# A three-stage attention and MLP kernel: two unrolled loops rolled up, a load moved behind other loads, and two copies moved one place ahead

## The reference

```python
# q, k, v: (8, 8, 576, 64), float32
scores = scale * np.matmul(q_c, k_c.transpose(0, 1, 2, 4, 3))     # in chunks of 64 tokens
attn = np.exp(scores - np.max(scores, axis=-1, keepdims=True))
attn = attn / (np.sum(attn, axis=-1, keepdims=True) + 1e-09)
x = np.matmul(attn, v_c)                                          # then (4608 tokens, 512)
h = x @ w_in_a;  r = np.maximum(h, 0.0);  y = (r * r) @ w_out_a   # first MLP: 512 -> 2048 -> 512
h = y @ w_in_b                                                    # second MLP, same sizes
g = np.where(h >= 1, h, np.where(h <= -1, 0.0, (h + 1) ** 2 / 4))
out = g @ w_out_b
```

## Time and profile before

| | us |
|---|---|
| median of 3 runs | 1613.38 (1612.52 to 1613.61) |
| the profiled execution's own time | 1612.52 |
| its span in the profile | 1610.7 |
| PE busy (matmuls) | 1599.8, 99% of the span |
| DVE busy | 1069.9, 66% |
| ACT busy | 628.8, 39% |
| POOL busy | 229.3, 14% |

### The profile page before, as it was taken

One profiled execution on the slowest core, in us unless ns is written; L12 is line 12 of the kernel. 1 busy time (PEld: TensorE's weight loads), 2 busy tenths in 40 slices (PEclk: granted clock), 3 DMA queues, 4 the chain that ended last, 5 costly groups with the idle time before them and its releaser, 6 DMA issues.

```text
span 1610.7 us, 27313 instructions
## 1 busy us (share of the span) xinstructions
PE 1599.8 (99%) x10446; PEld 1375.7 (85%) x10446; DVE 1069.9 (66%) x2125; ACT 628.8 (39%) x1495; POOL 229.3 (14%) x282
## 2 busy tenths in 40 slices
PE   8999999999999999999999999999999999999999
PEld 6888888888888888888888889999999999999998
DVE  4778776666767766653124577777777777776865
ACT  5554444444344444443552233323233323233322
POOL 5640000000000000000787500000000000000000
PEclk9999999999999999999999999999999999999999
DMA  9532121112111121210554353534353534344341
GB/s 196 136 89 60 34 66 41 53 40 67 40 27 53 40 67 29 64 40 29 179 159 157 105 157 105 158 105 141 95 157 105 157 106 134 102 130 132 105 131 53
DMA packets 179503, 154.84 MB, mean 96 GB/s; under 512 B 117153, under 2 KB 133537, under 8 KB 177073
## 3 DMA queue, kind: packets, MB, share of 16 engines
q0 software_dynamic: 38688, 83.96, 17.3%
q1 hardware_dynamic: 138032, 68.50, 15.5%
q10 hardware_dynamic: 2656, 0.66, 0.2%
HBM read 125.83 MB, written 27.26 MB: 95 GB/s over the span
## 4 chain that ended last, share of the span: by engine, by line
PE 98%; DMA 1%; DVE 0%; issue 0%; ACT 0%; POOL 0%; SPq 0%
PE banks L605 27%; PE banks L677 25%; PE banks L681 24%; PE banks L650 20%; PE banks L732 1%; PE banks L744 1%; DMA stage<-in_moe_w_in_dram 0%; DMA shared<-in_k_dram 0%; PE banks L720 0%; PE banks L616 0%; DVE prob_sum L1187 0%; DVE x_t_split L1120 0%; DVE score_max L1161 0%; POOL shared L499 0%; SPq L391 0%
## 5 line engine op out<-in xcount | busy, mean ns | idle before, releaser
L605 PE MATMUL banks<-x_t_split,w_in_split 128*128 128x512 f32 x1908 | 455.4, 389 | 0.0
L605 PEld LDWEIGHTS banks<-x_t_split,w_in_split 128*128 128x128 f32 x1908 | 358.1, 188 | 74.2
L677 PE MATMUL banks<-hidden_split,w_out_split 128*128 128x512 f32 x1728 | 417.8, 391 | 0.0
L681 PE MATMUL banks<-w_out_split,hidden_split 128*128 128x512 f32 x1728 | 406.3, 390 | 0.0
L677 PEld LDWEIGHTS banks<-hidden_split,w_out_split 128*128 128x128 f32 x1728 | 322.8, 188 | 67.8 <-issue 0.3
L681 PEld LDWEIGHTS banks<-w_out_split,hidden_split 128*128 128x128 f32 x1728 | 320.4, 188 | 63.8
L1267 DVE TENSOR_TENSOR hidden_split<-banks,hidden_split 128x512 fp32r<-128x512 f32 x144 | 99.6, 692 | 220.6 <-ACT banks L972 219.6
L1341 DVE TENSOR_TENSOR hidden_raw<-banks,hidden_raw 128x256 f32<-128x256 f32 x448 | 178.1, 422 | 100.1 <-PE banks L650 92.9
L967 ACT ACTIVATE banks<-banks 128x512 f32<-128x512 f32 x144 | 84.6, 588 | 376.1 <-PE banks L605 374.9
L1051 ACT ACTIVATE hidden_relu<-hidden_raw 128x512 f32<-128x512 f32 x128 | 80.9, 632 | 334.6 <-DVE hidden_raw L1341 234.5
L650 PE MATMUL banks<-x_sums_split,w_in_split 128*128 128x256 f32 x1536 | 195.5, 283 | 0.7 <-DVE hidden_raw L1341 0.7
(11 more groups left out here) (99 smaller groups left out, 1053.8 us busy)
## 6 DMA issues: line engine op xcount, KB each, us to landing
w_in_split<-w_in_sums_split POOLq DMA_DIRECT2D x64, 1024.0 KB, 5.4
mlp_out_t<-stage SPq DMA_DIRECT2D x9, 1024.0 KB, 3.9
v_and_probs_t<-mlp_out_t SPq DMA_DIRECT2D x9, 1024.0 KB, 7.1
shared<-in_q_dram SPq DMA_DIRECT2D x68, 128.0 KB, 2.9
shared<-in_k_dram SPq DMA_DIRECT2D x68, 128.0 KB, 3.1
v_and_probs_t<-in_v_dram SPq DMA_DIRECT2D x66, 128.0 KB, 3.1
w_in_sums_split<-shared POOLq DMA_DIRECT2D x16, 512.0 KB, 2.9
out_dram<-stage SPq DMA_DIRECT2D x8, 1024.0 KB, 5.0
```

The lines of the kernel that those rows point to most:

```text
L605: last = nc.tensor.matmul(h_ps[:, bank, :], w_in[:, kt, w, cols], x_t[:, par, x, kt, :], start=(kt == 0 and w == HI and x == HI), stop=(kt ...
L677: last = nc.tensor.matmul(acc[:, j, :], w_out[:, of_w, w, cols], hid[:, half, x, :], start=first, stop=end)
L681: last = nc.tensor.matmul(acc[:, j, :], hid[:, half, w, cols], w_out[:, of_w, x, :], start=first, stop=end)
```

## The change

There are four edits.

- **SP:** the six raw weight units 10 to 15 are now loaded before x of tile 10 and no longer behind it. The two waits that stand ahead of `load_x` move with it.
- **ACT and DVE:** of the eight tiles of pairs, 11 to 16 become a loop of three rounds of two tiles; 10 and 17 stay written out. The waits inside are worked out in registers.
- **DVE:** in the first pair of each tile of pairs, `copy_acc` moves ahead of both LO subtractions.

```diff
@@ sync @@
                 if f == FT:
                     store(TILES, mid[TILES - 1])
+            for u in range(FT // 2 + 2, UNITS):
+                load_raw_w(u)
             sp.wait_ge(stored, DMA * TILES)
             sp.wait_ge(x_lo, GROUPS * (TILES + 1))
             load_x(TILES + 1)
-            for u in range(FT // 2 + 2, UNITS):
-                load_raw_w(u)
             tile_of_pairs(TILES + 1)
@@ scalar; the same on vector @@
-            for t in range(TILES + 1, END):
-                tile_of_pairs(t, t % 2)
+            tile_of_pairs(TILES + 1, 0)
+            with act.Fori(TILES + 2, END - 1, 2) as t:
+                tile_of_pairs(t, 1)
+                tile_of_pairs(t + 1, 0)
+            tile_of_pairs(END - 1, 1)
@@ vector, tile_of_pairs @@
+                    if i == 0:
+                        copy_acc(t)
                     for half in range(2):
-                        if half == 1 and i == 0:
-                            copy_acc(t)
                         if goes_on and half == 1 and i in QUARTER_STEPS:
```

More of the change, by code:

```diff
@@ L1413, in _ @@
             tile(TILES, 1, 1, False)
-            for t in range(TILES + 1, END):
-                tile_of_pairs(t, t % 2)
+            tile_of_pairs(TILES + 1, 0)
+            with dve.Fori(TILES + 2, END - 1, 2) as t:
+                tile_of_pairs(t, 1)
+                tile_of_pairs(t + 1, 0)
+            tile_of_pairs(END - 1, 1)
             dve.wait_ge(stored, DMA * (END - 1))
```

## The result

| | before | after |
|---|---|---|
| median, us | 1613.38 (5 runs, 1612.17 to 1613.67) | 1621.39 (5 runs, 1621.26 to 1623.01) |
| profiled execution, us | 1612.52 | 1620.91 |
| its span, us | 1610.7 | 1619.0 |

The ratio after to before (of the means of the runs) is 1.0055, with a 95% interval of 1.004 to 1.0069. The change makes the kernel slower by 6.5 to 11.1 us; the medians are 8.0 apart.

A forecast was written before the change was run, and what follows sets the result against it. PE was taken to bound the kernel, busy 99% with 0.7 us of waiting to win. Terms 3.2 (x) + 0.2 (copies) + 1.8 (branches) = 5.2 us took 1612.52 to 1617.7; 0.9 for the median gave 1618.6, range 1616.1 to 1621.6.

The forecast's parts named there:

- the clock: Rival, chance 0.10: PE's clock falls in the tile 9 stall, one slice at half clock adds 2.7 us: 1621.3.
- the branches: DVE's loop branch, taken twice: 3.0 us from branch to work, PE stalls about 0.9 us each, 1.8 in all.
- The load of x: Tile 9, ahead of `down` of slice 9: x for tile 10 goes out at about 894.8, PE stalls 3.2 us.
- The landing: Load of x for tile 10: lands in 5.1 us, the short end of nine loads taking 5.1 to 9.0.
- From ACT's quarter to PE: Tile 9: chain from ACT's cast of the quarter through DVE and ACT to `down` of slice 9, 4.40 us.
- The raw loads: SP's queue: POOL sets their pace, so issuing them earlier in the program wins nothing.
- its own signs of being wrong: No PE wait in tile 9, granted clock below full behind it, or waits inside the loop's tiles would refute the forecast.
- The rule on instruction fetch: Loop branches: targets outside two pages of 256 instructions need a DMA fetch; by the rule alone, no 1.8 us.
- The copies: First pair of tile 10: `first_copied` comes later and PE loses 0.2 us once; tiles 11 to 17 cost nothing.
- Only x is late: Rival, chance 0.22: x stalls PE in tile 9 but the loops cost nothing; 3.4 us, 1616.8.
- the two with x in time: Rivals, no stall in tile 9: loops free, 1613.6, chance 0.05; or branches cost 1.8, 1615.4, chance 0.06.
- the slow landing: Rival, chance 0.07: x lands in 7.1 to 9.0 us, 2.0 to 3.9 us more: 1620.6 to 1622.5.

The follow-up runs named there:

- e2: Kernel before with SP's edit, but the load of x between raw units 14 and 15: 0.00 us in the trace, ratio 0.9999.
- e1: Kernel before with SP's edit alone, x of tile 10 behind raw units 10 to 15: +6.86 us in the trace, ratio 1.0037.
- e4: Kernel before with SP's edit and the load of x held until POOL has split unit 13: +7.99 us in the trace.
- e14: Kernel before with the load of x just ahead of raw unit 15, on the same signal of POOL: +4.39 us in the trace.
- e15: Kernel before with SP's edit alone, a repeat of e1 without a change: +6.53 us in the trace.
- e3: Kernel before with the load of x sent after two of POOL's four sums of unit 13, unit 15 behind it: +1.79 us in the trace.
- e13: e1 plus five unread matmuls on PE in the standstill of tile 9: +4.20 us against the kernel before, in the trace.
- e16: Changed kernel with the load of x back ahead of the raw loads: +2.85 us against the kernel before, ratio 1.0018.
- e9: Kernel before with only DVE's copies moved ahead of both LO subtractions: +0.26 us in the trace.
- e7: Kernel before with DVE's tiles 11 and 12 in a loop of a single round, branch never taken: -0.04 us in the trace.
- e10: Kernel before with DVE's loop alone, rounds ending between the second pair's two LO subtractions: +0.02 us in the trace, ratio 1.0005.
- e11: Kernel before with DVE's copies of tile 10 behind the first two additions of its second pair: -0.92 us, ratio 0.9992.

## Why the prediction was right and wrong

The direction was right, and so were the places of three of the four new losses. The size was not: 5.2 us forecast, 8.47 in the trace, 8.9 by the ratio. Of the 3.3 us between forecast and trace, 1.7 are the clock, 0.8 the branches and 0.7 the wait for x. That the median lies just inside the range, whose top is 1621.6, is luck: the top came from a rival that priced the fall of the clock at 2.7, and the fall cost 1.7 here, with 1.5 from terms that the sum had too small.

- **The load of x.** The mechanism held link by link. I put it at 3.2, and it was 3.88. The landing was mis-sized: I took the shortest of nine landings, 5.1, and it was 5.71. From ACT's quarter to PE it was 4.46 against 4.40.
- **The raw loads.** Right: they went out at the old pace, and e2 shows that having five units ahead of x is free.
- **The clock.** This is the step that failed. I had it as a rival with one chance in ten, because the trace before had no PE that stood still for 3.2 us, and took it as an alternative to the forecast. But absence from a trace in which the case never arises is no evidence against it. Given the standstill that I forecast myself, the fall was the likely thing: it came in each of the five runs with 2.9 us or more in tile 9 (the change, e1, e4, e14, e15), at 1.5 to 2.9 us. The Trainium skill says that idle gaps between bursts of matmuls bring the clock down ("TensorE: Matmul & The Clock Gate", section "HAM oscillation"), and these five traces agree. The fall should have stood in the sum, as soon as rows gave a standstill. The prediction had it among its own signs of being wrong.
- **The branches.** The delay of the sequencer, 2.8 and 3.1 us, was that of the earlier trace rows, and the waits of PE were 0.98 and 1.22, where 0.9 was forecast for each. I priced the wait and not the delay. From start to start PE lost 1.20 and 1.43, so 2.63 and not 1.8.
- **The rule on instruction fetch** ("Runtime: NRT & Kernel Launch", section "Instruction fetch mechanics") names a window of two pages of 256 instructions. In the runs, rounds of 241 and 321 returned in 0.2 us, rounds of 369 to 431 in 2.4 to 3.6, with a packet of instructions behind the branch. The mechanism agrees; as a size, two pages were not enough for rounds that would fit in them. The plain count in the prediction, 333 and 415, was too low, since it left out the instructions that only wait: it should have been 391 and 431.
- **The copies.** 0.24, forecast 0.2, once and in tile 10 alone.
- **The rivals.** *Only x is late*, the two with x in time and the slow landing are out. The forecast and the clock came true together, which I had not allowed: with the clock's 1.7 in the sum it would have been 1620.3, and with what the traces gave for landing and branches 1621.8.

## What to carry to other kernels

When a forecast has the bound engine stand still for some microseconds, put the fall of its clock into the sum: here it added 40 to 70% to a standstill of 3 to 4 us, and nothing to the one of 1.8 in e3. A load may wait until its consumer's slack is used up and not one queue entry longer, so compute its landing against that consumer before it is moved behind loads that another engine paces. A loop whose round is so long that its start is fetched again (369 instructions and more here, and not 321) costs 2.4 to 3.6 us at each taken branch; put the end of the round where the engine has that much slack, and it is free.

## What the runs showed of the hardware

**The clock also falls at the start of the program, in some executions.** In the first 40 us PE waits for ACT by an amount that differs from one execution to the next (none in the kernel before's, 0.7 to 2.2 us in the others). In four of the traces (e3, e13, e15, e16; waits of 1.8 to 2.2 us) the granted clock fell behind it; e3's row of this time, and the matmuls:

```profile
34.77 0.69 PE L746 MATMUL banks<-shared 64*64 64x64 f32 x32 [2.24 <-ACT shared L924]
35.39 4.60 PE L607 MATMUL banks<-x_t_split,w_in_split 128*128 128x512 f32 x12
```

```profile
36.00:40.00 4.00, 4.00 (x12) 3.14 (x12) 3.82 (x10) 1.14 (x2) 2.69 (x4) 0.62 0.83 175
```

In e9 the same wait was 2.05 us long, and the twelve matmuls behind it kept their length, 3.02. So near two microseconds it can go either way. In four others (e4, e7, e10, e11) the clock was at its lower level from 18 to 20 us, behind waits of only 1.0 and 0.8 us. The kernel before has such waits there too, 0.9 and 0.8, and kept its full clock. So the length of one wait doesn't settle it. A fall at 36 us adds 1.6 us to an execution, which is larger than several of the effects studied here; that is why the table above measures from a point behind it.

**A wait of PE costs more than it is long.** From start to start the waits in tile 9 and at the branches cost 0.16 to 0.23 us more than the idle time in the row's bracket (3.72 and 3.88; 0.98 and 1.20; 1.22 and 1.43; in e16 1.18 and 1.41).
